# A fused convolution and two-layer network on one core: channels laid out over partitions, so that VectorE turns 32x32 blocks in place of TensorE's transposes

## The chip, the cores and the metric

The kernel runs on one core of a Trainium2 chip. The metric is the device time of one execution in microseconds (us), as the median of several runs. TensorE is called PE here, VectorE DVE, ScalarE ACT, GpSimd POOL, and SyncE SP, as the profile calls them.

## What is computed

```python
# x: 4 x 4096 x 192, weight_gen: 4 x 4096 x 8 x 7, w_in: 192 x 2048, w_out: 2048 x 192
w = softmax(weight_gen, axis=-1)                    # 7 taps for each token and each of 8 heads
x_unf = windows of 7 tokens (the token and the 6 before it, zeros before a sequence's start)
y = einsum('bshk,bskhg->bshg', w, x_unf)            # 24 channels per head, 192 in all
h = y.reshape(16384, 192) @ w_in
g = where(h >= 1, h, where(h <= -1, 0, (h + 1)**2 / 4))
out = g @ w_out
```

## The kernel before

**Tiling.** The 16384 tokens are cut into 128 runs of 128 tokens, one run on each partition. A group is 4 tokens of each run, 512 tokens; there are 32 groups, in 16 pairs (`pair`, `b`). The group of two buffers is `b`. The first pair and the last are written out, the 14 between are a loop.

**The convolution.** For a group, `softmax` makes the taps `tap_w` in six DVE steps with an exponential on ACT between the second and the third, and `convolve` makes 7 products and 6 sums of 768 elements on each partition into `conv`. For the first group DVE convolves, for the others POOL, two groups ahead of PE's use. 64 of the 192 channels are written twice (line 350), so that the second transpose gives them in both halves of the partitions.

**The turn.** PE needs channels on partitions. `turn(pair, b, part)` (line 598) transposes the next group's `conv` into a PSUM slot with four products by the identity; part 0 is channels 0 to 127, part 1 the other 64, twice. ACT copies a turned part out rounded to fp32r (`xt_high`, `xt_rest`), and DVE subtracts the rounded one from the slot (`xt_low`, lower half of `xt_rest`). `TURN_AFTER` says after which of the 16 tiles of a group the parts of the next one are turned.

**The network.** A group has 16 tiles `n` of 128 hidden units. `hidden` (line 617) adds up five products of 512 columns in one of four PSUM slots: the weights and the activations are both split into a rounded and a remaining part. ACT makes `half_relu` and `square`, DVE the `gate`, ACT rounds it (`gate_high`), DVE makes the rest (`gate_low`), and three tiles later (`LAG`) PE's `outputs` (line 637) adds eight products to the accumulators `acc`. At tile 2 of the next group the accumulators are copied, summed and stored.

**The start.** The weights are loaded in four chunks and split by ACT (`in_high`, `out_high`) and DVE (`in_low`, `out_low`), partly before the loop, partly at the tiles of the first group named in `LOWS_AFTER`.

**What sets the order.** All of it is written out by hand: each engine runs its own list in order and waits on semaphores. SP issues nearly all transfers: for each group `store` (two groups back), then `reload` (two groups ahead, once `conv` of the group that used the buffer is done).

Of the kernel before, what the change touches and what calls it, by code (L numbers as in the profile page):

```python
# [19 lines left out]
P = 128  # L20
SLOTS = 4
# [5 lines left out]
OUT_HIGHS_AFTER = {2: 2, 4: 3}  # L27
# [4 lines left out]
TURN_AFTER = (3, 8)  # L32
FIRST_TURNS_AFTER = ((12, 14), (5, 10))
EVICT_AT = 2

# [4 lines left out]
def build(nc, x, weight_gen, w_in, w_out, out):  # L40
# [5 lines left out]
    RUN = B * S // P  # L46
    TOK = 4
    GT = TOK * P
    GROUPS = RUN // TOK
    PAIRS = GROUPS // 2  # L50
    PAD = K - 1
    R = D - P
    HK = H * K
    CT = NT // W_CHUNKS
    CW = FF // W_CHUNKS
    USES = NT + 2
    SEQ_PARTS = S // RUN
    assert R == 64 and (2 * USES) % SLOTS == 0 and NT % W_CHUNKS == 0 and GROUPS % 2 == 0

    x_runs = x.rearrange("b s d -> (b s d)").rearrange("(p r) -> p r", p=P)  # L60
    w_runs = weight_gen.rearrange("b s h k -> (b s h k)").rearrange("(p r) -> p r", p=P)
    out_runs = out.rearrange("t d -> (t d)").rearrange("(p r) -> p r", p=P)
    w_out_tiles = w_out.rearrange("(n p) d -> p n d", p=P)

    with ExitStack() as ctx:
# [7 lines left out]
        x_in = [sb(f"x_in{b}", [P, TOK + PAD, D]) for b in range(2)]  # L73
        gen_in = [sb(f"gen_in{b}", [P, TOK * H, K]) for b in range(2)]
        tap_w = [sb(f"tap_w{b}", [P, TOK, H, K]) for b in range(2)]
        gen_max = sb("gen_max", [P, TOK * H])
        gen_shift = sb("gen_shift", [P, TOK * H, K])
        gen_exp = sb("gen_exp", [P, TOK * H, K])
        gen_sum = sb("gen_sum", [P, TOK * H])
        gen_sum_eps = sb("gen_sum_eps", [P, TOK * H])  # L80
        gen_inv = sb("gen_inv", [P, TOK * H])

        conv = [sb(f"conv{b}", [P, TOK, D + R]) for b in range(2)]
        tap = [sb(f"tap{b}", [P, TOK, D]) for b in range(3)]
        ident = sb("ident", [P, P])
# [27 lines left out]
        in_loaded = [sem(f"in_loaded{c}") for c in range(W_CHUNKS)]  # L113
        out_w_loaded = [sem(f"out_w_loaded{c}") for c in range(W_CHUNKS)]
        x_padded = sem("x_padded")
        ident_done = sem("ident_done")
# [12 lines left out]
        turned = sem("turned")  # L129
        turned_high_done = sem("turned_high_done")  # L130
        turned_low_done = sem("turned_low_done")
# [34 lines left out]
        def turn_after(pair, b):  # L166
            if is_first(pair):
                return FIRST_TURNS_AFTER[b]
            return () if b == 1 and is_last(pair) else TURN_AFTER

        def uses(pair, b):
            order = []
            for n in range(NT):
                order.append(("tile", n))
                order += [("turn", part) for part, at in enumerate(turn_after(pair, b)) if at == n]
            return order

        def tile_slot(pair, b, n):
            return slot[(USES * b + uses(pair, b).index(("tile", n))) % SLOTS]

        def turn_slot(pair, b, part):

            if b == 0 and is_first(pair):
                return slot[2 + part]
            pair, b = before(pair, b)
            return slot[(USES * b + uses(pair, b).index(("turn", part))) % SLOTS]
# [15 lines left out]
        def slot_free(eng, pair, b, use):  # L202


            held = uses(pair, b).index(use) - SLOTS
            if held < 0 and b == 0 and is_first(pair):
                if held >= -2:
                    eng.wait_ge(turned_low_done, held + 3)
                return
            if held < 0:  # L210
                pair, b = before(pair, b)
            kind, k = uses(pair, b)[held]
            if kind == "tile":
                wait(eng, gate_low_done, pair, 2 * NT, NT * b + k + 1)
            else:
                wait(eng, turned_low_done, pair, 4, 2 * (b + 1) + k + 1)

# [6 lines left out]
        def is_edge(pair):  # L224
            return isinstance(pair, int) and pair == 1

        EDGE_X = 1 + 2 * B
        block = ctx.enter_context(nc.Block())

        @block.sync  # L230
        def _(sp):
            def load_gen(pair, b):
                at = (at_pair(pair) * 2 + b) * (TOK * HK)
                sp.dma_start(gen_in[b][:].rearrange("p t k -> p (t k)"),
                             w_runs[:, bass.ds(at, TOK * HK)]).then_inc(gen_loaded[b], 16)

            def load_x(pair, b):

                at = ((at_pair(pair) * 2 + b) * TOK - PAD) * D
                sp.dma_start(x_in[b][:].rearrange("p t d -> p (t d)"),  # L240
                             x_runs[:, bass.ds(at, (TOK + PAD) * D)]).then_inc(x_loaded[b], 16)

            def load_edge_x(b):

                before = PAD - b * TOK
                half = SEQ_PARTS // 2
                flat = x_in[b][:].rearrange("p t d -> p (t d)")
                sp.dma_start(flat[:, before * D:], x_runs[:, 0:(TOK + PAD - before) * D]
                             ).then_inc(x_loaded[b], 16)
                for s in range(B):  # L250
# [22 lines left out]

            load_x(0, 0)
            load_in(0)
            load_in(1)
            load_out(0)
            load_gen(0, 1)
            load_in(2)
# [405 lines left out]
```

## Time and profile before

| what | value |
|---|---|
| median of 3 runs | 1238.05 us (1237.85 to 1238.25) |
| the profiled execution | 1238.25 us, its span 1236.5 us |
| granted TensorE clock, mean | 0.999 of full speed |
| PE busy | 1208.8 us, 98% |
| DVE, ACT, POOL busy | 819.2, 897.5, 696.5 us |
| HBM traffic | 38.77 MB read, 12.58 MB written |

The span is the time from the first to the last instruction; the execution takes 1.75 us more. Busy shares are averages over a start in which PE has little to do and 31 groups that are alike.

### The profile page before, as it was taken

To read this page: it belongs to the slowest core of one execution; us is meant where nothing else is said; L and a number is where in the kernel's file an instruction comes from. 1 tells how busy PE (TensorE), PEld (TensorE's weight loads), DVE (VectorE), ACT (ScalarE), POOL (GpSimd) and SP (SyncE) were. 2 spreads that over 40 slices of the span, in tenths; PEclk is the share of its full clock that TensorE was granted. 3 is DMA by queue.
4 is the path that set the end of the run, shared out by engine and by line. 5 is a ranking of instruction groups with operands and counts; after the bars stand their busy time and mean duration, and the time that the engine had idled before them with its cause. 6 is when DMAs were issued, how large, how long until landed. Compare 5 with 4: busy or idle time off the path is not lost.

```text
span 1236.5 us, 21147 instructions
## 1 busy us (share of the span) xinstructions
PE 1208.8 (98%) x6932; PEld 1092.3 (88%) x6932; DVE 819.2 (66%) x1434; ACT 897.5 (73%) x1773; POOL 696.5 (56%) x450
## 2 busy tenths in 40 slices
PE   3899999999999999999999999999999999999998
PEld 3789999999999999999999999999999999999997
DVE  7966666666666666666666666666666666666665
ACT  4677777777777777777777777777777777777776
POOL 1975775546765456765557755567654567655500
PEclk9999999999999999999999999999999999999999
DMA  7111101111011111011111011110011110110000
GB/s 225 36 50 49 39 11 48 48 49 48 13 35 48 48 48 48 0 48 48 48 48 38 10 48 48 48 48 16 32 48 48 48 48 0 48 48 13 14 14 13
DMA packets 17667, 51.60 MB, mean 42 GB/s; under 512 B 2040, under 2 KB 8308, under 8 KB 17648
## 3 DMA queue, kind: packets, MB, share of 16 engines
q1 hardware_dynamic: 17504, 51.25, 12.7%
q8 instruction: 10, 0.16, 0.1%
q10 hardware_dynamic: 144, 0.11, 0.0%
q14 instruction: 9, 0.07, 0.0%
HBM read 38.77 MB, written 12.58 MB: 42 GB/s over the span
## 4 chain that ended last, share of the span: by engine, by line
PE 93%; POOL 4%; DVE 2%; DMA 0%; ACT 0%; issue 0%; POOLq 0%; DVEq 0%
PE slot L617 46%; PE acc L637 44%; PE slot L598 2%; POOL tap L329 2%; POOL conv L348 1%; DMA gen_in<-in_weight_gen 0%; DVE tap L329 0%; POOL tap L348 0%; POOL x_in L373 0%; POOL conv L352 0%; DVE conv L348 0%; POOL conv L329 0%; POOL conv L350 0%; DVE gate_low L510 0%; ACT gate_high L407 0%
## 5 line engine op out<-in xcount | busy, mean ns | idle before, releaser
L637 PE MATMUL acc<-out_parts,gate_high 128*128 128x384 f32 x2048 | 616.0, 357 | 4.9 <-DVE gate_low L510 4.8
L510 DVE TENSOR_TENSOR gate_low<-slot,gate_high 128x512 fp32r<-128x512 f32 x512 | 353.5, 690 | 400.5 <-ACT gate_high L407 400.3
L396 ACT ACTIVATE half_relu<-slot 128x512 f32<-128x512 f32 x512 | 307.7, 601 | 289.0 <-PE slot L617 288.9
L637 PE MATMUL acc<-out_parts,gate_low 128*128 128x192 f32 x2048 | 513.3, 251 | 0.5 <-DVE gate_low L510 0.5
L637 PEld LDWEIGHTS acc<-out_parts,gate_high 128*128 128x128 f32 x2048 | 384.4, 188 | 26.8 <-DVE gate_low L510 8.1
L637 PEld LDWEIGHTS acc<-out_parts,gate_low 128*128 128x128 f32 x2048 | 389.8, 190 | 17.8 <-DVE gate_low L510 0.7
L504 DVE SCALAR_TENSOR_TENSOR slot<-slot,square 128x512 f32<-128x512 f32 x512 | 352.8, 689 | 0.1
L402 ACT ACTIVATE square<-half_relu 128x512 f32<-128x512 f32 x512 | 325.2, 635 | 0.0
L407 ACT ACTIVATE gate_high<-slot 128x512 fp32r<-128x512 f32 x512 | 304.0, 594 | 27.9 <-DVE slot L504 27.7
L329 POOL TENSOR_TENSOR conv<-x_in,tap_w 128x768 f32<-128x768 f32 x31 | 47.9, 1546 | 460.0 <-DVE tap_w L494 459.9
L329 POOL TENSOR_TENSOR tap<-x_in,tap_w 128x768 f32<-128x768 f32 x186 | 288.8, 1560 | 0.0
L348 POOL TENSOR_TENSOR conv<-conv,tap 128x768 f32<-128x768 f32 x124 | 230.6, 1860 | 0.0
L617 PE MATMUL slot<-xt_high,in_main_high 128*128 128x512 f32 x512 | 211.6, 413 | 0.7 <-DVE in_rest_low L540 0.3
L617 PE MATMUL slot<-xt_low,in_main_high 128*128 128x512 f32 x512 | 202.1, 395 | 0.0
L617 PE MATMUL slot<-xt_rest,in_rest_high 128*128 128x512 f32 x512 | 201.3, 393 | 0.2 <-DVE xt_rest L523 0.2
L617 PE MATMUL slot<-xt_high,in_main_low 128*128 128x512 f32 x512 | 201.1, 393 | 0.0
L617 PE MATMUL slot<-xt_rest,in_rest_low 128*128 128x512 f32 x512 | 199.1, 389 | 0.0
L617 PEld LDWEIGHTS slot<-xt_rest,in_rest_low 128*128 128x128 f32 x512 | 96.2, 188 | 23.0
L617 PEld LDWEIGHTS slot<-xt_rest,in_rest_high 128*128 128x128 f32 x512 | 96.0, 188 | 22.7 <-DVE xt_rest L523 0.5
L617 PEld LDWEIGHTS slot<-xt_low,in_main_high 128*128 128x128 f32 x512 | 96.1, 188 | 21.6 <-DVE xt_low L519 0.5
L617 PEld LDWEIGHTS slot<-xt_high,in_main_low 128*128 128x128 f32 x512 | 97.7, 191 | 0.1
L617 PEld LDWEIGHTS slot<-xt_high,in_main_high 128*128 128x128 f32 x512 | 96.2, 188 | 1.5 <-issue 0.8
(41 smaller groups left out, 492.7 us busy)
## 6 DMA issues: line engine op xcount, KB each, us to landing
x_in<-in_x SPq DMA_DIRECT2D x30, 960.0 KB, 5.1
out<-out_sb SPq DMA_DIRECT2D x32, 384.0 KB, 2.5
gen_in<-in_weight_gen SPq DMA_DIRECT2D x31, 112.0 KB, 2.3
out_raw<-in_moe_w_out SPq DMA_DIRECT2D x4, 384.0 KB, 10.6
in_main<-in_moe_w_in SPq DMA_DIRECT2D x4, 256.0 KB, 6.1
in_rest<-in_moe_w_in SPq DMA_DIRECT2D x8, 128.0 KB, 6.5
x_in<-in_x SPq DMA_DIRECT2D x1, 768.0 KB, 4.1
x_in<-in_x SPq DMA_DIRECT2D x1, 384.0 KB, 3.4
```

What stands on the lines that cost most here:

```text
L329: ops.tensor_tensor(dst[:, :, 0:D].rearrange("p t (h c) -> p t h c", h=H), x_in[b][:, k:k + TOK, :].rearrange("p t (h c) -> p t h c", h=H) ...
L348: ops.tensor_tensor(to, conv[b][:, :, 0:D], tap[k % 3][:], ALU.add).then_inc(step_sem, 1)
L396: nc.scalar.activation(half_relu[n % 2][:], tile_slot(pair, b, n)[:], ACT.Relu, scale=0.5, bias=0.5).then_inc(relu_done, 1)
L402: nc.scalar.activation(square[n % 2][:], half_relu[n % 2][:], ACT.Square).then_inc(square_done, 1)
L407: nc.scalar.activation(gate_high[n % 4][:], tile_slot(pair, b, n)[:], ACT.Copy).then_inc(gate_high_done, 1)
L504: nc.vector.scalar_tensor_tensor(h[:], h[:], 1.0, square[n % 2][:], ALU.max, ALU.min).then_inc(gate_done, 1)
L510: nc.vector.tensor_tensor(gate_low[n % 4][:], tile_slot(pair, b, n)[:], gate_high[n % 4][:].bitcast(F32), ALU.subtract).then_inc(gate_low_ ...
L598: ins = nc.tensor.transpose(dst[:, i * P:(i + 1) * P], conv[b][:, i, part * P:(part + 1) * P], ident[:])
L617: ins = nc.tensor.matmul(tile_slot(pair, b, n)[:], w[:, units], xt[b][:], start=(j == 0), stop=(j == len(products) - 1))
L637: ins = nc.tensor.matmul(dst, stationary, moving, start=(n == 0 and j == 0), stop=(n == NT - 1 and j == 1))
```

## The change

The tokens are now 32 runs ("lanes") of 512 tokens, and a partition is one lane and one quarter of the channels: quarter `q` of lane `r` is partition 32`q` + `r`. A group is 16 tokens of each lane. A partition holds 48 of the 192 channels: 32 "main" ones and 16 "rest". DVE's 32x32 block transpose (`turn_main`) of the main ones gives 4 x 32 channels on 128 partitions. Of the rest, ACT writes the rounded part and POOL (for the first group DVE) what remains beside it, in `rest_parts`, and a second block transpose (`turn_rest`) gives both on 128 partitions. `main_turn` is split by ACT and POOL into `xt_high` and `xt_low`. `rest_turn` is copied to `xt_rest` by a transfer from SBUF to SBUF that SP issues (for the first group by ACT). No channel is written twice any more. The rows of `w_in` are loaded in the order of the new partitions.

Loads change their shape. `x` and `weight_gen` are read in four transfers each, one for a quarter, in runs of 48 floats (192 B) and 14 floats (56 B), where before a partition's 7,680 B and 896 B were contiguous in HBM; at the start the `x` of the first group is loaded from ACT's queue. ACT's splits of the later weight chunks move into the first group (`HIGHS_AFTER`), PE's slots are used by tiles alone, and the second to fifth product of a hidden tile stand in another order.

```diff
-OUT_HIGHS_AFTER = {2: 2, 4: 3}
+HIGHS_AFTER = {1: ("out", 1), 3: ("in", 6), 4: ("in", 7), 5: ("out", 2), 7: ("out", 3)}
-TURN_AFTER = (3, 8)
-FIRST_TURNS_AFTER = ((12, 14), (5, 10))
+MAIN_AFTER, REST_AFTER = 3, 8
+FIRST_MAIN_AFTER, FIRST_REST_AFTER = (11, 7), (13, 10)
...
+        def load_gen(eng, pair, b, q):
+            lanes = slice(q * LANES, (q + 1) * LANES)
+            eng.dma_start(gen_in[b][lanes].rearrange("p (t h) k -> p t (h k)", h=HQ),
+                          w_quads[q][:, bass.ds(group_at(pair, b) * STEP, STEP), :]
+                          ).then_inc(gen_loaded[b], 16)
+        def load_x(eng, pair, b, q):
+            lanes = slice(q * LANES, (q + 1) * LANES)
+            eng.dma_start(x_in[b][lanes],
+                          x_quads[q][:, bass.ds(group_at(pair, b) * STEP - PAD, STEP + PAD), :]
+                          ).then_inc(x_loaded[b], 16)
+        def load_main(eng, c):
+            eng.dma_start(in_main[:, cols], w_in_quads[:, 0:MAIN, cols]).then_inc(main_loaded[c], 16)
...
+            def copy_rest(pair, b):
+                wait(sp, rest_turned, pair, 2, b + 1)
+                sp.dma_start(xt_rest[b][:].bitcast(F32), rest_turn[:]).then_inc(xt_rest_copied, 16)
             def body(pair):
                 for b in range(2):
                     if not is_first(pair):
                         store(pair - 1, b)
                     if not is_last(pair):
                         reload(pair + 1, b)
+                    if has_next(pair, b):
+                        copy_rest(*after(pair, b))
...
-            ops.tensor_tensor(conv[b][:, :, D:D + R], tap[K % 3][:, :, P:D],
-                              tap[(K - 1) % 3][:, :, P:D], ALU.add).then_inc(step_sem, 1)
...
+            def lows(pair, b):
+                wait(pool, rest_high_done, pair, 2, b + 1)
+                rest_low(nc.gpsimd, b).then_inc(rest_low_done, 1)
+                wait(pool, xt_high_done, pair, 2, b + 1)
+                wait(pool, hidden_done, pair, 2 * NT, NT * (b - 1))
+                main_low(nc.gpsimd, b).then_inc(xt_low_done, 1)
...
                         convolve(pool, nc.gpsimd, pair + 1, b)
+                        lows(pair + 1, b)
...
-            def turned_top(pair, b, part):
-                wait(act, turned, pair, 4, 2 * b + part + 1)
-                dst = (xt_high, xt_rest)[part][b]
-                nc.scalar.activation(dst[:], turn_slot(pair, b, part)[:], ACT.Copy
+            def rest_high(pair, b):
+                nc.scalar.activation(rest_parts[:, :, 0:REST], conv[b][:, :, MAIN:CH], ACT.Copy
+            def main_high(pair, b):
+                nc.scalar.activation(xt_high[b][:], main_turn[:], ACT.Copy).then_inc(xt_high_done, 1)
...
+            for half in range(4):
+                in_high(half)
             out_high(0)
-            turned_top(0, 0, 0)
-            turned_top(0, 0, 1)
+            rest_high(0, 0)
+            main_high(0, 0)
+            act.wait_ge(rest_turned, 1)
+            nc.scalar.activation(xt_rest[0][:], rest_turn[:], ACT.Copy).then_inc(first_xt_rest_done, 1)
             exponent(0, 1)
-            out_high(1)
+            in_high(4)
+            in_high(5)
...
-            def turned_rest(pair, b, part):
-                    nc.vector.tensor_tensor(xt_low[b][:], src[:], xt_high[b][:].bitcast(F32),
-                                            ALU.subtract).then_inc(turned_low_done, 1)
+            def turn_main(pair, b):
+                nc.vector.transpose(main_turn[:], by_block(conv[b][:])[:, :, :, 0:MAIN]
+            def turn_rest(pair, b):
+                nc.vector.transpose(rest_turn[:], by_block(rest_parts[:].bitcast(F32))
...
             convolve(dve, nc.vector, 0, 0)
+            dve.wait_ge(rest_high_done, 1)
+            rest_low(nc.vector, 0).then_inc(first_rest_low_done, 1)
+            turn_main(0, 0)
+            turn_rest(0, 0)
+            dve.wait_ge(xt_high_done, 1)
+            main_low(nc.vector, 0).then_inc(first_xt_low_done, 1)
             in_low(0)
             in_low(1)
             softmax(0, 1, 1)
-            turned_rest(0, 0, 0)
-            turned_rest(0, 0, 1)
...
-            def turn(pair, b, part):
-                for i in range(TOK):
-                    ins = nc.tensor.transpose(dst[:, i * P:(i + 1) * P],
-                                              conv[b][:, i, part * P:(part + 1) * P], ident[:])
```

PE's list, at a tile of the looped groups after which a part was turned. Before:

```order
L617 MATMUL slot<-xt_rest,in_rest_high 128x512
L617 MATMUL slot<-xt_rest,in_rest_low 128x512
L598 MATMUL slot<-ident,conv 128x128 x4
L149 REGISTER_ALU
L637 MATMUL acc<-out_parts,gate_high 128x384
```

The same place in the changed kernel:

```order
L689 MATMUL slot<-xt_high,in_main_high 128x512
L689 MATMUL slot<-xt_low,in_main_high 128x512
L689 MATMUL slot<-xt_rest,in_rest_high 128x512
L689 MATMUL slot<-xt_high,in_main_low 128x512
L689 MATMUL slot<-xt_rest,in_rest_low 128x512
L173 REGISTER_ALU
L709 MATMUL acc<-out_parts,gate_low 128x192
```

The four products of line 598 are gone from it, and the five of the tile stand in another order.

SP's list at the start of the program (shapes are those of the SBUF side). Before:

```order
L240 DMA x_in<-in_x 128x1920
L264 DMA in_main<-in_moe_w_in 128x512
L267 DMA in_rest<-in_moe_w_in 64x512 x2
L264 DMA in_main<-in_moe_w_in 128x512
L267 DMA in_rest<-in_moe_w_in 64x512 x2
L271 DMA out_raw<-in_moe_w_out 128x4x192
L234 DMA gen_in<-in_weight_gen 128x224
L264 DMA in_main<-in_moe_w_in 128x512
```

In the changed kernel:

```order
L233 DMA gen_in<-in_weight_gen 32x16x14 x4
L246 DMA in_main<-in_moe_w_in 128x1x512
L253 DMA in_rest<-in_moe_w_in 16x512 x4
L275 DMA out_raw<-in_moe_w_out 128x4x192
L246 DMA in_main<-in_moe_w_in 128x1x512
L253 DMA in_rest<-in_moe_w_in 16x512 x8
L233 DMA gen_in<-in_weight_gen 32x16x14 x4
L240 DMA x_in<-in_x 32x22x48 x4
L246 DMA in_main<-in_moe_w_in 128x1x512
L253 DMA in_rest<-in_moe_w_in 16x1024 x8
```

The third chunk of `in_main` now stands behind the whole of the second group's `gen_in` and `x_in`, eight transfers of short runs.

## Rows read from the trace of the kernel before

**Rows 1.** The page: busy time, and the chain that ended last.

```profile
PE 1208.8 (98%) x6932; PEld 1092.3 (88%) x6932; DVE 819.2 (66%) x1434; ACT 897.5 (73%) x1773; POOL 696.5 (56%) x450
PE slot L617 46%; PE acc L637 44%; PE slot L598 2%; POOL tap L329 2%; POOL conv L348 1%; DMA gen_in<-in_weight_gen 0%; DVE tap L329 0%; POOL tap L348 0%; POOL x_in L373 0%; POOL conv L352 0%; DVE conv L348 0%; POOL conv L329 0%; POOL conv L350 0%; DVE gate_low L510 0%; ACT gate_high L407 0%
```

**Rows 2.** PE's timeline in two groups: start, duration (us), line, operation.

```profile
507.37 0.41 PE L617 MATMUL slot<-xt_high,in_main_high 128*128 128x512 f32 x1
...
521.09 0.41 PE L617 MATMUL slot<-xt_high,in_main_high 128*128 128x512 f32 x1
...
524.59 0.60 PE L598 MATMUL slot<-ident,conv 128*128 128x128 f32 x4
...
562.07 0.60 PE L598 MATMUL slot<-ident,conv 128*128 128x128 f32 x4
```

**Rows 3.** Groups by form: xcount | busy us, mean ns | idle before.

```profile
L348 POOL TENSOR_TENSOR conv<-conv,tap 128x768 f32<-128x768 f32 x124 | 230.6, 1860 | 0.0
L598 PE MATMUL slot<-ident,conv 128*128 128x128 f32 x256 | 38.3, 273 | 1.5 <-POOL conv L352 0.8 <-DVE conv L352 0.5 <-DVE gate_low L510 0.2
L350 POOL TENSOR_TENSOR conv<-tap 128x256 f32<-128x256 f32 x31 | 22.8, 737 | 2.4
L519 DVE TENSOR_TENSOR xt_low<-slot,xt_high 128x512 fp32r<-128x512 f32 x32 | 21.8, 680 | 0.0
L414 ACT ACTIVATE xt_high<-slot 128x512 fp32r<-128x512 f32 x32 | 18.9, 590 | 1.6 <-PE slot L598 1.6
```

**Rows 4.** POOL's and DVE's timeline about one group's convolution.

```profile
500.21 1.55 POOL L329 TENSOR_TENSOR conv<-x_in,tap_w 128x768 f32<-128x768 f32 x1 [15.39 <-DVE tap_w L494]
520.59 1.86 POOL L352 TENSOR_TENSOR conv<-tap 128x768 f32<-128x768 f32 x1
528.10 0.68 DVE L519 TENSOR_TENSOR xt_low<-slot,xt_high 128x512 fp32r<-128x512 f32 x1
```

**Rows 5.** DVE's and PE's timeline for the tile of 507.37 us.

```profile
512.15 0.69 DVE L510 TENSOR_TENSOR gate_low<-slot,gate_high 128x512 fp32r<-128x512 f32 x1 [0.99 <-ACT gate_high L407]
515.40 0.33 PE L637 MATMUL acc<-out_parts,gate_high 128*128 128x384 f32 x1
```

**Rows 6.** The start: timeline of DVE and PE.

```profile
6.27 0.39 DVE L479 TENSOR_REDUCE gen_max<-gen_in 128x32 f32<-128x224 f32 x1 [6.27 <-DMA gen_in<-in_weight_gen]
9.13 0.96 DVE L329 TENSOR_TENSOR conv<-x_in,tap_w 128x768 f32<-128x768 f32 x1
20.02 0.95 DVE L352 TENSOR_TENSOR conv<-tap 128x768 f32<-128x768 f32 x1
24.18 0.40 PE L617 MATMUL slot<-xt_rest,in_rest_low 128*128 128x512 f32 x1
```

**Rows 7.** Windows of start and first group: busy us, PEclk, DMA share, GB/s.

```profile
0.00:22.36 22.36, 5.31 (x28) 4.91 (x28) 15.29 (x23) 7.65 (x13) 0.78 (x8) 1.00 0.92 264
22.36:65.21 42.85, 37.09 (x192) 30.13 (x193) 39.35 (x55) 28.78 (x54) 38.24 (x24) 1.00 0.18 51
```

**Rows 8.** DVE's timeline in the first group, beside POOL at work.

```profile
36.08 0.37 DVE L479 TENSOR_REDUCE gen_max<-gen_in 128x32 f32<-128x224 f32 x1
48.11 1.64 DVE L494 TENSOR_TENSOR tap_w<-gen_exp,gen_inv 128x224 f32<-128x224 f32 x1
50.88 1.82 DVE L540 TENSOR_TENSOR in_main_low<-in_main,in_main_high 128x512 fp32r<-128x512 f32 x1
```

**Rows 9.** DMA, windows 0:40, 531:531.4, 1235:1236.4: packets, MB, 16 engines' share.

```profile
q10 hardware_dynamic: 144, 0.11, 0.9%
...
q1 hardware_dynamic: 5, 0.00, 0.7%
...
q1 hardware_dynamic: 79, 0.19, 35.5%
```

**Rows 10.** DMA issues: KB each, median us from issue to landing.

```profile
out<-out_sb SPq DMA_DIRECT2D x32, 384.0 KB, 2.5
gen_in<-in_weight_gen SPq DMA_DIRECT2D x31, 112.0 KB, 2.3
```

More of the change, by code:

```diff
@@ L162, in is_last, with main_after, rest_after, has_next @@
             return isinstance(pair, int) and pair == PAIRS - 1
[L166 to L186, printed above, removed]
+        def main_after(pair, b):
+            return FIRST_MAIN_AFTER[b] if is_first(pair) else MAIN_AFTER
+        def rest_after(pair, b):
+            return FIRST_REST_AFTER[b] if is_first(pair) else REST_AFTER
+        def has_next(pair, b):
+            return not (b == 1 and is_last(pair))
+        def tile_slot(n):
+            return slot[n % SLOTS]
         def before(pair, b):
@@ L200, in wait_conv @@
                 wait(eng, conv_done, pair, 2, at)
[L202 to L216, printed above, removed]
         def at_pair(pair):
@@ L230, in _ @@
         @block.sync
         def _(sp):
[L232 to L241, printed above, removed]
@@ new lines, in wait_rest_low, with wait_xt_low, rest_low @@
+        def wait_rest_low(eng, pair, b):
+            if b == 0 and is_first(pair):
+                eng.wait_ge(first_rest_low_done, 1)
+            else:
+                wait(eng, rest_low_done, pair, 2, b)
+        def wait_xt_low(eng, pair, b):
+            if b == 0 and is_first(pair):
+                eng.wait_ge(first_xt_low_done, 1)
+            else:
+                wait(eng, xt_low_done, pair, 2, b)
+        def rest_low(ops, b):
+            return ops.tensor_tensor(rest_parts[:, :, REST:2 * REST], conv[b][:, :, MAIN:CH],
+                                     rest_parts[:, :, 0:REST].bitcast(F32), ALU.subtract)
@@ L423, in take_cross, with in_high @@
                                          ).then_inc(cross_copied, 1)
[L425 to L426 removed]
+            for q in range(QUADS):
+                load_x(act, 0, 0, q)
+            load_rest(act, 0, 0)
             exponent(0, 0)
[L429 removed]
+            def in_high(half):
+                c, rest = divmod(half, 2)
                 cols = slice(c * CW, (c + 1) * CW)
[L431 to L433 removed]
+                if rest:
+                    act.wait_ge(rest_loaded[min(c, 2)], 16 * 2 * QUADS)
+                else:
+                    act.wait_ge(main_loaded[c], 16)
+                raw, high = ((in_main, in_main_high), (in_rest, in_rest_high))[rest]
+                nc.scalar.activation(high[:, cols], raw[:, cols], ACT.Copy).then_inc(in_high_done, 1)
             def out_high(c):
@@ L588, in _ @@
         def _(pe):
-            def turn(pair, b, part):
-                if not (b == 0 and is_first(pair)):
-                    slot_free(pe, *before(pair, b), ("turn", part))
-                if part == 0:
-                    wait_conv(pe, pair, b)
-                dst = turn_slot(pair, b, part)
-                for i in range(TOK):
-                    ins = nc.tensor.transpose(dst[:, i * P:(i + 1) * P],
-                                              conv[b][:, i, part * P:(part + 1) * P], ident[:])
-                ins.then_inc(turned, 1)
```

303 lines of the change are left out of this document (173 added, 130 removed).

## The prediction

> **What bounds the kernel now.** I read the busy times and the chain of waits first [rows 1]: PE is busy for 1208.8 us of a span of 1236.5, and the chain runs almost wholly through its products, 46% in the hidden tiles, 44% in the outputs and 2% in the transposes of line 598. Then the timeline of PE far from both ends [rows 2]: two hidden tiles six apart start at 507.37 and 521.09 us, so a tile takes 13.72 / 6 = 2.287 us, and the same transposes come back after 562.07 - 524.59 = 37.48 us. Sixteen tiles are 36.59 us, so the two turned parts cost a group 0.89 us of PE's time. The view by groups gives 256 transposes of 273 ns, 38.3 us in all [rows 3]; they overlap, so 0.89 a group is the price on the path.
>
> The start has other limits. The first tile ends at about 24.6 us (24.18 + 0.40), behind the load of `gen_in` (the softmax waits for it until 6.27), the softmax (convolution from 9.13) and the convolution (until 20.97) [rows 6]. The DMA engines are 92% busy there at 264 GB/s [rows 7]. The first group then takes 42.85 us, though its three missing outputs make it shorter than the others: DVE is busy for 39.35 of them [rows 7], since it splits the weights. So the time is: 65.21 us to the end of the first group, 30 groups of 37.48, the last, which turns nothing, of 36.59, and 10.3 us that remain of the span behind it. The profiled execution took 1238.25 us, 1.75 more than its span and 0.2 more than the median of 1238.05, which is nothing here: a difference of 0.2% is about what a measurement of this kernel can tell from none.
>
> **Steady groups: what is removed.** Without line 598 a group is 36.59 us. 30 x 0.89 = 26.7 us.
>
> **Steady groups: what is added.** DVE loses two subtractions of 512 columns a group at 0.68 us [rows 3] and gains two block transposes of 512 columns. No row shows a block transpose. The nearest is the subtraction of as many columns, 0.68; I take 0.7. It may also have to wait for POOL: beside POOL's work DVE's `tap_w` took 1.64 and `in_main_low` 1.82 us, while `gen_max` took 0.37 [rows 8]; the usual `in_main_low` of as many columns would be 0.68, so the wait is up to 1.2 us. `turn_main` falls where POOL is idle, `turn_rest` (tile 8) where POOL convolves. Bounds: 0.4 (the 0.37 of `gen_max`, a DVE row of half the columns) to 4 x 0.68 + 1.2 = 3.9 us, if the turn took four passes. What covers it: DVE is idle 0.99 us in every tile, and the `gate_low` of the tile that started at 507.37 ends at 512.84 while PE uses it at 515.40 [rows 5], 2.56 us later. A turn is free up to 0.99 + 2.56 = 3.5 us.
>
> The Trainium skill (VectorE: DVE Perf Modes, The three transpose paths) gives 311 ns for a 128x128 bf16 transpose on VectorE. Four of these would be an estimated 1.24 us for ours, also under cover; no run here shows it yet.
>
> ACT's two copies of a turned part, 0.59 each [rows 3], become one of 512 and one of 256 columns. POOL loses the doubled channels (0.74) and gains `rest_low` of the same size (0.74) and `main_low` (512 of 768 columns at 1.86, 1.24 us). It is idle 15.39 us before each convolution, waiting for the taps of tile 7 [rows 4]; the lows run at tiles 3 to 5 of that gap. The convolution ended at 522.45 (520.59 + 1.86) and the turn's DVE work began at 528.10 [rows 4]: 5.6 us in hand. I take nothing for all of it.
>
> SP now waits for `rest_turned` (tile 8) before it issues the copy; behind it stand `store` and `reload`. The reload is then issued 11 tiles (25 us) before DVE asks for `gen_in` at tile 3 of the next group. The copy has 8 tiles (18 us) to land; a transfer of 384 KB lands in 2.5 us, one of 112 KB in 2.3 [rows 10], so 2.4 is the copy's. Nothing.
>
> **What a short run costs.** A group's loads are 4 x 32 x 16 = 2048 runs of 56 B and 4 x 32 x 22 = 2816 of 192 B, 4864 packets, 304 for each of 16 engines. Prices from the DMA windows [rows 9]: 5 semaphore packets took 0.7% of 16 x 0.4 us, 9 ns each; those of the 144 of queue 10 that carry 896 B took 0.9% of 16 x 40 us less 16 x 9 ns over 128, 44 ns each; 63 of 3072 B, 35.5% of 16 x 1.4 us less the same, 124 ns each. A line through the last two gives 18 ns for 192 B and 13 for 56 B, 15 in the mean: the low end. The high end is a flat 44. I take 35, nearer to the flat one, for short reads scattered in HBM. A group's loads are then 10.6 us of a 36.6 us group: hidden.
>
> The Trainium skill (DMA: Bandwidth & Descriptors, Specifications) asks for at least 512 B and says that below it an engine reads, modifies and writes. It speaks against this change and gives no price; no packet of data under 512 B is in this trace.
>
> **The start.** `gen_in` and `x_in` of the first group come on two queues that share the engines. A transfer's fixed part is about 2 us (2.3 less 8 x 44 ns) and the first issue stands at 0.75. `gen_in` lands at 0.75 + 2 + 256 x 0.035 = 11.7 us; the softmax's 2.86 us (9.13 - 6.27) put the convolution at 14.6, **+5.5**. Two halves in place of the last sum and the doubled channels: -0.25. Then DVE does `rest_low` (0.4), both turns (1.4) and `main_low` (0.7), `in_low` (1.2), and the first tile ends about 4.5 us after the convolution where it was 3.6: **+0.9**. ACT has two splits of 0.6 before the loop instead of one: I take **+0.8**, in_main and in_rest together being longer than the one they replace. These need the third weight chunk: behind 2.75 + 10.6 us stand 1.44 MB of weights at 264 GB/s (5.5), the second group's loads (10.6) and 0.79 MB more (3.0), 32.4 us, then 1.2 of splitting: **+1.5** beyond what ACT would have reached. The first copy has only tiles 13 to 16: DVE ends a gate 3.8 us after its tile began (512.15 less its 0.99 us of idle time, against 507.37 [rows 5]), then come the turn (0.7) and issue and transfer (0.6 + 2.4), 7.5 us. PE wants it in the third product of the third tile on, 3 x 2.287 + 0.46 = 7.3. In the first group DVE runs late by a split or so: **+1.0**. The two turns of the first group go: -0.9. Together +8.6.
>
> **Sum:** 65.2 + 8.6 + 31 x 36.59 + 10.3 = 1218.4, plus 1.75: **1220 us**.
>
> With 608 short packets per engine on the way to the loop, each ns of price is 0.6 us once ACT waits for weights: 15 ns gives 1213, 44 ns gives 1226.
>
> **Rivals.**
>
> *Late weights, slower than before.* From 31 ns on, the start costs 608 t - 12.5 us (t in us), and it eats the 26.7 saved at t = 65 ns. The mean over all startup packets of this trace is no guide, since they are long. At 90 ns, twice the 896 B row, the time is 1254; against it stands that price falls with size between the three rows. A packet above 120 ns would also fill a group. Chance 0.08.
>
> *Fewer engines.* `load_main` and `store` now have a side whose outermost dimension is 4. If that decides how many engines share a transfer, a store's 32 packets per engine instead of 8 take 24 x 124 ns = 3.0 us more on the last store, and three chunks of `in_main` at 24 more packets of about 90 ns (between the 44 and 124 rows) are 6.5 us later; both add: 1220 + 9.5 = 1229 us. Chance 0.27.
>
> The Trainium skill (DMA: Bandwidth & Descriptors, Why a DMA increments its semaphore by 16 and not by 1) states this rule: the largest number up to 16 that divides both sides' slowest dimension. Every large transfer of this trace has 64 or 128 rows on both sides, so no row bears it out or refutes it.
>
> *DVE becomes the bound.* If a turn beside POOL takes the 3.9 us of the upper bound, PE waits 0.4 us in 31 groups: 1232. Slower than before from 4.2 us on. Chance 0.05.
>
> *The saving is smaller because PE waited for something else anyway.* Against: in the rows of the page PE is at 98%, and the removed products stand between tiles with no gap. That the transposes stay is excluded by PE's list. Chance 0.02, 1236.
>
> **Chances.** The likeliest, short packets between 15 and 50 ns, all 16 engines: 0.58, with 1211 to 1229. Faster by over 0.2% is that, fewer engines and most of the DVE case: 0.89. Slower: late weights and a piece of the DVE case, 0.09. Same: 0.02. The range goes from 1210 (low price, nothing lost at the first copy) to 1234 (fewer engines and a price of 43 ns).
>
> **What the next profile would show.** Right: no PE idle time inside steady groups, tiles of 2.287 us, 36.6 a group; DVE's transposes near 0.7 us, the second up to 1.9; POOL's wait for the taps about 13 us; the first tile ending near 30 us. Wrong: PE waiting for `xt_rest` each group (the copy is late), DVE `gen_max` waiting for `gen_in` in the loop (short packets over 65 ns), ACT waiting for `in_main` before the loop for more than 5 us (price, or fewer engines), `gate_low` named as PE's releaser (DVE).

## The result and the profile after

The changed kernel takes 1222.03 us (median; 1221.9 to 1223.1) against 1238.13 measured beside it (1237.85 to 1238.25), a ratio of 0.9872 (0.9855 to 0.9889). It is 16.1 us faster, 1.3%, and 2 us from the predicted 1220. The agreement is partly luck: three errors of 3 to 7 us cancel in it, as the sections below take apart.

The page of the changed kernel, in the same views as [rows 1]: the span, the busy times, and (the fourth line from its section 4) the chain that ended last.

```profile
span 1220.2 us, 21278 instructions
...
PE 1185.1 (97%) x6676; PEld 1066.4 (87%) x6676; DVE 841.3 (69%) x1436; ACT 901.4 (74%) x1774; POOL 731.9 (60%) x473
...
PE 93%; DVE 2%; SPq 2%; ACT 1%; DMA 1%; issue 0%; DVEq 0%
```

PE has 256 instructions fewer (6932 to 6676), the transposes of line 598. It is still the bound, at 97%, but SP's issuing now has 2% of the chain, at the start. The new loads read less (24.62 MB instead of 38.77) in many more packets (171,875 instead of 17,667); the main DMA queue's share of the 16 engines rose from 12.7% to 18.5%.

PE's timeline, the first product of chosen tiles (start, duration, line, operation), as in [rows 2]: the first tile of group 1, the third product of its first tile, the first tile of group 2, tiles 1 to 4 of a later group (583.91 to 590.92), the first tile of the last group, and the last tile of all.

```profile
66.65 0.41 PE L689 MATMUL slot<-xt_high,in_main_high 128*128 128x512 f32 x1
...
67.65 0.50 PE L689 MATMUL slot<-xt_rest,in_rest_high 128*128 128x512 f32 x1 [0.35 <-DMA xt_rest<-rest_turn]
...
104.11 0.41 PE L689 MATMUL slot<-xt_high,in_main_high 128*128 128x512 f32 x1
...
583.91 0.41 PE L689 MATMUL slot<-xt_high,in_main_high 128*128 128x512 f32 x1
...
586.20 0.41 PE L689 MATMUL slot<-xt_high,in_main_high 128*128 128x512 f32 x1
...
588.50 0.39 PE L689 MATMUL slot<-xt_high,in_main_high 128*128 128x512 f32 x1
...
590.92 0.41 PE L689 MATMUL slot<-xt_high,in_main_high 128*128 128x512 f32 x1
...
1169.42 0.41 PE L689 MATMUL slot<-xt_high,in_main_high 128*128 128x512 f32 x1
...
1203.91 0.41 PE L689 MATMUL slot<-xt_high,in_main_high 128*128 128x512 f32 x1
```

The first tiles of group 1, of group 2 and of the last group, and the last tile, in the kernel before, which [rows 2] do not hold:

```profile
65.21 0.41 PE L617 MATMUL slot<-xt_high,in_main_high 128*128 128x512 f32 x1
...
103.87 0.41 PE L617 MATMUL slot<-xt_high,in_main_high 128*128 128x512 f32 x1
...
1191.76 0.41 PE L617 MATMUL slot<-xt_high,in_main_high 128*128 128x512 f32 x1
...
1226.27 0.41 PE L617 MATMUL slot<-xt_high,in_main_high 128*128 128x512 f32 x1
```

With the two spans these starts cut the 16.3 us of span into four parts:

| part | before | after | difference | predicted |
|---|---|---|---|---|
| to the first tile of group 1 | 65.21 | 66.65 | +1.4 | +8.6 |
| 30 groups, per group | 37.55 | 36.76 | -23.8 in all | -26.7 |
| first to last tile of the last group | 34.51 | 34.49 | 0.0 | 0 |
| start of the last tile to the end of the span | 10.23 | 16.29 | +6.1 | 0 |

The predicted +8.6 holds 1.0 for the first copy of `rest_turn`; what that copy cost was paid in group 1. Group 1 is longer than the 29 behind it in both kernels: 38.66 us against 37.51 before, 37.45 against 36.73 after. Before, one of its turns waited 0.8 us for POOL's convolution [rows 3]; after, its first tile waits for the copy.

The rows 583.91 to 590.92 show a loss inside the groups: tiles come every 2.29 and 2.30 us, and then one takes 2.42. The views by form and by wait tell more: the groups that answer to [rows 3], and the waits of POOL, PE's loader and SP (us in all, times, longest).

```profile
L586 DVE STREAM_TRANSPOSE main_turn<-conv 128x512 f32<-128x512 f32 x32 | 22.5, 702 | 0.0
L596 DVE STREAM_TRANSPOSE rest_turn<-rest_parts 128x512 f32<-128x512 f32 x32 | 22.4, 701 | 0.0
```

```profile
POOL conv L352 <- DVE tap_w L559: 187.3, 29, 6.5
POOL rest_parts L397 <- ACT rest_parts L461: 158.5, 31, 8.2
PEld acc L709 <- DVE out_sb L603: 8.5, 28, 0.3
PEld slot L689 <- DMA xt_rest<-rest_turn: 0.8, 1, 0.8
SPq L331 <- DMA out<-out_sb: 7.9, 1, 7.9
```

DVE's transpose is as quick as forecast, the copy of `rest_turn` is waited for once, at the first copy, and SP's last wait, for the last store, is 7.9 us. In the kernel before it was

```profile
SPq L310 <- DMA out<-out_sb: 2.0, 1, 2.0
```

### The profile page after: what moved, and what is told of

It reads as the page before. It is cut to its first block, busy times and chain, and to the rows that moved or that the text cites. A ratio compares the mean times of both kernels' runs of the same rounds, so it can differ in the third digit from the quotient of the medians.

```text
span 1220.2 us, 21278 instructions
## 1 busy us (share of the span) xinstructions
PE 1185.1 (97%) x6676; PEld 1066.4 (87%) x6676; DVE 841.3 (69%) x1436; ACT 901.4 (74%) x1774; POOL 731.9 (60%) x473
## 2 busy tenths in 40 slices
DMA packets 171875, 45.59 MB, mean 37 GB/s; under 512 B 160848, under 2 KB 162896, under 8 KB 171856
## 3 DMA queue, kind: packets, MB, share of 16 engines
q1 hardware_dynamic: 168848, 44.68, 18.5%
HBM read 24.62 MB, written 12.58 MB: 30 GB/s over the span
## 4 chain that ended last, share of the span: by engine, by line
PE 93%; DVE 2%; SPq 2%; ACT 1%; DMA 1%; issue 0%; DVEq 0%
PE slot L689 48%; PE acc L709 46%; DVE slot L569 1%; SPq L253 1%; DMA in_rest<-in_moe_w_in 1%; DVE gate_low L575 1%; SPq L233 1%; ACT gate_high L451 0%; DVE out_parts L620 0%; SPq L240 0%; DMA xt_rest<-rest_turn 0%; SPq L246 0%; ACT square L446 0%; DVE gen_sum_eps L552 0%; DVE gen_shift L546 0%
## 5 line engine op out<-in xcount | busy, mean ns | idle before, releaser
L397 POOL TENSOR_TENSOR rest_parts<-conv,rest_parts 128x256 fp32r<-128x256 f32 x31 | 22.8, 737 | 158.5 <-ACT rest_parts L461 158.5
```

What stands on the lines that cost most here:

```text
L397: return ops.tensor_tensor(rest_parts[:, :, REST:2 * REST], conv[b][:, :, MAIN:CH], rest_parts[:, :, 0:REST].bitcast(F32), ALU.subtract)
```

## The experiments

Three questions stood after the result: what made the tail 6 us longer, what took back 3 us of the steady saving, and why the start cost so little. Where two medians of different kernels are subtracted below, the changed kernel's 1222.03 is the base unless said otherwise. The diffs are cut: the semaphore counts that go with an edit are left out.

### The last store

The store's HBM side is now `j r g e`, with 4 outermost. The view of the DMA queues over the last stretch (packets, MB, share of 16 engines), 1226:1236.5 of the kernel before and 1210:1220.2 of the changed one, each with just one store in it:

```profile
q1 hardware_dynamic: 144, 0.39, 9.6%
```

```profile
q1 hardware_dynamic: 132, 0.39, 14.6%
```

Both carry 128 data packets of 3072 B. The others are semaphore packets, 16 before and 4 now: four engines took part. Their work is 0.146 x 16 x 10.2 = 23.8 us, 186 ns a packet, and 32 packets on each of four engines are 6.0 us. The data packets ran from 1212.50 to 1219.43, so 3.4 were under way at a time in the mean; before, they ran from 1234.50 to 1235.63, at 124 ns a packet 14 at a time. The Trainium skill (DMA: Bandwidth & Descriptors, Why a DMA increments its semaphore by 16 and not by 1) says that each engine taking part posts one semaphore write and that their number is the largest up to 16 that divides both sides' slowest dimension; the trace agrees, with 4 and 16.

**The store in four transfers of 32 partitions**, in the changed kernel:

```diff
-                sp.dma_start(out_steps[:, :, bass.ds(group_at(pair, b), 1), :],
-                             out_sb[b][:].rearrange("p t d -> p (t d)"))
+                for j in range(STEP // TOK):
+                    lanes = slice(j * LANES, (j + 1) * LANES)
+                    sp.dma_start(out_steps[j][:, bass.ds(group_at(pair, b), 1), :],
+                                 out_sb[b][lanes].rearrange("p t d -> p (t d)"))
```

> The changed kernel with each store of 384 KB issued as four transfers of 32 lanes (one for each of the four steps j) instead of one transfer whose HBM side has 4 as its outermost dimension. Theory (that outermost 4 lets only four DMA engines share the store): the last store lands in about 3 us instead of 8.7, plus up to 1.5 us for three more issues; the time falls by 4 to 6 us, to 1216 to 1218. Rival (the store is slow because its rows are scattered in HBM): nothing changes in the rows, so the time stays at 1222.

1216.81 us (1216.66 to 1217.05), 5.2 less. From the start of the last tile to the end of the span it is now 11.00 us in place of 16.29 (10.23 before the change); what is left of the difference, 0.8, is about what SP needs for four issues in place of one (1.71 us against 0.54). A packet is no quicker in the four transfers (208 ns in the mean); more of them run at a time. SP's last wait:

```profile
SPq L333 <- DMA out<-out_sb: 1.4, 1, 1.4
```

**The same HBM pattern alone, in the kernel before** (it writes each token's output to another place of `out`):

```diff
+                rows = out_runs.rearrange("(r j) e -> j r e", j=4)
-                sp.dma_start(out_runs[:, bass.ds(at, TOK * D)],
+                sp.dma_start(rows[:, :, bass.ds(at, TOK * D)],
```

> The kernel before with its store written with an HBM side of 4 x 32 rows, the order of the changed kernel's store, same rows of 3072 B and the same count; each output row goes to another place of the output, so the output is permuted. Theory (four engines): the last store lasts 6 us longer and the time is 1244. Rival (the changed kernel's end is longer for another reason): 1238.

1244.12 us (1243.94 to 1244.38), 1.005 of the kernel before (1.0033 to 1.0066), 6.0 slower. Its groups take 37.55 us as before, and the stretch behind the last tile's start grew from 10.23 to 16.32. So the pattern alone accounts for the whole tail. It also holds up what queues behind it, as the landing times of `gen_in` (last number) show; here they cost nothing, since the loads have a group's time in hand.

```profile
gen_in<-in_weight_gen SPq DMA_DIRECT2D x31, 112.0 KB, 8.4
```

In the kernel before that was 2.3 [rows 10].

### The steady groups

DVE adds up the accumulators (`out_sb`) at the first tiles of a group, and PE's first `outputs` of that group, at tile 3, needs them free. DVE's and PE's timeline there:

```profile
588.69 0.69 DVE L575 TENSOR_TENSOR gate_low<-slot,gate_high 128x512 fp32r<-128x512 f32 x1 [0.99 <-ACT gate_high L451]
589.29 1.14 DVE L603 TENSOR_TENSOR out_sb<-acc,out_cross 128x192 f32<-128x192 f32 x4
...
589.70 0.44 PE L709 MATMUL acc<-out_parts,gate_high 128*128 128x384 f32 x1
```

The sums stand behind a `gate_low` on DVE and begin at 589.29, and the first product into `acc` follows at 589.70, about when the first of the four sums is done; this tile is the one of 2.42 us, 0.13 longer than its neighbours. In the kernel before, the four transposes after tile 3 stood between the hidden tile and these products, 0.44 us in which the wait was hidden.

**Four products of 128 columns put back after tile 3**, on the identity, into the slot of the next tile, their results unused:

```diff
                         hidden(pair, b, n)
+                        if n == 3 and has_next(pair, b) and not (b == 0 and is_first(pair)):
+                            wait(pe, gate_low_done, pair, 2 * NT, NT * b + n + 1 - SLOTS + 1)
+                            for i in range(TOK):
+                                nc.tensor.transpose(tile_slot(n + 1)[:, i * P:(i + 1) * P], warm[:], warm[:])
```

> The changed kernel with four transposes of a constant 128x128 tile put back on PE behind hidden tile 3, where the first turned part stood, in 30 groups; their result is overwritten. Theory (in the kernel before these products hid part of PE's wait for the accumulators to be summed, so that only part of their 0.43 us was a price): a group grows by 0.43 less the wait of 0.15 to 0.2, so 30 x 0.25 = 7.5 us, to 1229 to 1230. Rival (the wait has nothing to do with it): 30 x 0.43 = 12.9 us, to 1235.

1231.72 us (1231.49 to 1231.81), 9.7 more. This lies between the two values forecast, 1229 to 1230 and 1235, nearer to the theory's. **The same after tile 8** (`n == 8`), where the old kernel turned its second part:

> The same four transposes behind hidden tile 8, where PE waits for nobody. Both theories: 30 x 0.43 = 12.9 us, to 1235. The difference to the run with them behind tile 3 is the wait that they cover there: 5 us by the theory, 0 by the rival.

1235.38 us (1235.30 to 1237.02), 13.35 more. The profiled execution is the one of 1237.02; what it took longer lies ahead of group 1, which starts there at 68.30. The waits of PE's loader in the first of the two:

```profile
PEld acc L713 <- DVE gate_low L579: 8.5, 4, 6.4
PEld slot L693 <- ACT xt_high L471: 1.7, 1, 1.7
```

and in the second:

```profile
PEld acc L713 <- DVE out_sb L607: 8.5, 28, 0.3
```

At tile 3 the wait for `out_sb` is gone; at tile 8 it stands as in the changed kernel. The two differ by 3.66 us, less than the 5 I expected. Per group, between the first tiles of group 1 and of the last, they take 37.085 and 37.202 us against 36.759. So four products cost 0.443 where they cover nothing, and 0.326 at tile 3: the cover was worth **0.117 us a group**, 3.5 in all. The wait's row says 8.5 / 28 = 0.30 a time; that is time of the loader, most of it under a running product.

**The sums ahead of the gate on DVE**, nothing else changed:

```diff
-                        if n > 0:
-                            gate_rest(pair, b, n - 1)
-                        ...
                         if n == EVICT_AT and not (b == 0 and is_first(pair)):
                             sum_outputs(*before(pair, b))
+                        if n > 0:
+                            gate_rest(pair, b, n - 1)
+                        ...
```

> The changed kernel with DVE's four sums of the accumulators ahead of gate_low at tile 2 of a group instead of behind it. Theory (PE waits 0.1 to 0.2 us in each group for the sums, since the transposes that covered them are gone): the sums come 0.35 us earlier, the wait goes, and the time falls by 3 to 4.5 us, to 1218. Rival (the run with products behind tile 3 was shorter for another reason): 1222, or more if gate_low then comes late.

1218.45 us (1218.30 to 1218.55), 3.6 less; groups of 36.642 us, 0.117 less, and PE's waits name `out_sb` no more. **The same edit in the kernel before**, as a control, since there the transposes should cover the wait:

> The same exchange in the kernel before, as a control. Theory (there the transposes cover the sums in 31 groups of 32): within 1 us of 1238. Rival (an earlier sum helps whatever stands on PE): 1234.

1237.81 us (1237.64 to 1238.15), 0.9998 of the kernel before (0.9989 to 1.0008): no change, and its groups take 37.55 us as before. That settles it. The price of the two turned parts, 2 x 0.443 = 0.887, less the lost cover of 0.117 is 0.77 a group, where 37.55 - 36.76 = 0.79 was measured.

### The start

ACT's timeline, its last DMA waits before the loop and its first `half_relu`:

```profile
27.54 0.63 ACT L490 ACTIVATE in_main_high<-in_main 128x512 fp32r<-128x512 f32 x1 [1.79 <-DMA in_main<-in_moe_w_in]
29.71 0.63 ACT L490 ACTIVATE in_rest_high<-in_rest 128x512 fp32r<-128x512 f32 x1 [1.53 <-DMA in_rest<-in_moe_w_in]
30.25 0.58 ACT L440 ACTIVATE half_relu<-slot 128x512 f32<-128x512 f32 x1
```

In the kernel before the first `half_relu` was at

```profile
25.28 0.58 ACT L396 ACTIVATE half_relu<-slot 128x512 f32<-128x512 f32 x1
```

so ACT entered the loop 5.0 us late, and 3.3 of it are the waits for the third weight chunk. But PE began its first tile at 22.73 (before: 22.36) and group 1 only 1.4 us later than before: the first group won back 3.5. The chain that ended last runs through SP's issues up to the last part of `in_rest`'s third chunk, and then through its load:

```profile
22.22 7.47 DMA in_rest<-in_moe_w_in
```

So three things stand ahead of this wait: the issues of so many transfers, the short runs, and how fast the weights land. **`in_main` in four transfers of 32 rows** asks whether the wait is another case of four engines:

```diff
-            eng.dma_start(in_main[:, cols], w_in_quads[:, 0:MAIN, cols])
+            for q in range(QUADS):
+                eng.dma_start(in_main[q * LANES:(q + 1) * LANES, cols], w_in_quads[q][0:MAIN, cols])
```

> The changed kernel with each chunk of in_main loaded in four transfers of 32 rows instead of one whose HBM side is 4 x 32. Theory (four engines carry it alone, and they hold up what is queued behind on them): chunk 3 of the weights, which ACT got 9 us after its issue, lands 4 us or less after it; eight more issues stand ahead of it on SP, some 4 us, so ACT's wait stays about as it is and the time is 1221 to 1224. Rival (the transfers are late only because SP issues them late): landing after issue does not change and the time grows by the issues, 1225 to 1227.

1219.74 us (1219.62 to 1219.93), 2.3 less and outside the 1221 to 1224 that I expected: I had left ACT's wait as it was, and it went. The issues and landings of the changed kernel:

```profile
out_raw<-in_moe_w_out SPq DMA_DIRECT2D x4, 384.0 KB, 9.7
...
in_rest<-in_moe_w_in SPq DMA_DIRECT2D x8, 64.0 KB, 5.4
```

and of this one, where both waits of ACT are gone and the first `half_relu` starts at 26.69:

```profile
out_raw<-in_moe_w_out SPq DMA_DIRECT2D x4, 384.0 KB, 4.8
...
in_rest<-in_moe_w_in SPq DMA_DIRECT2D x8, 64.0 KB, 2.8
```

The transfers *behind* `in_main` land in half the time after their issue although they weren't touched. They are there earlier in the trace's own time too: ACT's split of the first chunk of `in_rest` starts at 10.27 instead of 13.09, that of the second at 14.05 instead of 17.68. So `in_main`, on its four engines, had held up their parts on these engines. Group 1 starts at 64.20 instead of 66.65; the first group, from PE's first tile on, takes 41.48 us instead of 43.92.

**The third chunk issued ahead of the second group's short loads:**

```diff
+            load_main(sp, 2)
+            for half in range(2):
+                load_rest(sp, half, 2)
             for q in range(QUADS):
                 load_gen(sp, 0, 1, q)
             for q in range(QUADS):
                 load_x(sp, 0, 1, q)
-            load_main(sp, 2)
-            for half in range(2):
-                load_rest(sp, half, 2)
```

> The changed kernel with the third chunk of in_main and the rest of in_rest loaded ahead of the second group's gen_in and x_in on SP. Theory (ACT's waits for the third chunk, 1.8 and 1.5 us before its first relu, hold up the start): they go, the first relu comes 3 us earlier, and the time falls by 1.5 to 3 us, to 1219 to 1220.5, since DVE bounds the rest of the first group. Rival (DVE would have been late by as much anyway): 1222.

1221.45 us (1220.93 to 1221.52), 0.6 less. ACT's splits no longer wait and its first `half_relu` is at 28.29, but PE's first tile starts at 24.32 in place of 22.73: ACT waited 11.0 us instead of 7.9 for the first two chunks and came to `rest_parts` at 22.12 instead of 20.49. The first group takes 41.46 us. So the wait went as wholly as with `in_main` in four parts, and most of it came back ahead of the first tile; the expectation of 1.5 to 3 was wrong. Why the first two chunks land later was not tested.

**Long rows in the first pair**: its `x` and `weight_gen` are read as 4,224 B and 896 B contiguous on each partition (the first two groups then compute on other values).

```diff
+            if is_first(pair):
+                eng.dma_start(gen_in[b][lanes].rearrange("p a k -> p (a k)"),
+                              w_flat[:, q * STEP * HQ * K:(q + 1) * STEP * HQ * K])
+                return
...
```

> The changed kernel with the loads of x and weight_gen of the first two groups taken as one contiguous run for each partition, as many bytes and as many transfers; these two groups compute on other values than the reference's. It prices the short runs at the start. By the prediction (35 ns a packet, 600 packets an engine) 8 us of the start would go: 1214. By the trace of the changed kernel (15 to 20 ns a packet; first convolution at 9.5 us against 9.1) ACT's wait for chunk 3 shrinks by 3 us at most: 1219 to 1221.

1219.60 us (1218.94 to 1221.00), 2.4 less: all the short runs of the start cost together 2.4 us, with a wider spread than the other runs have. By the prediction's price of 35 ns it would have been 1214. PE's first tile starts at 21.81, 0.9 earlier, and the first group takes 41.44 us. These three edits differ, and each brings the first group from 43.92 to 41.4 or 41.5: each takes away by itself all that PE felt of ACT's late start. Their gains need not add, no run has two of them, and the wait can't be put down to one of the three causes. The price itself can be read in the loop, where nothing else moves. The changed kernel's DMA queues over 614:617:

```profile
q1 hardware_dynamic: 2326, 0.41, 74.3%
```

0.743 x 16 x 3.0 us over 2326 packets is **15.3 ns** each, for a mix of 56 and 192 B (176 B in the mean). And the start agrees: DVE's timeline,

```profile
6.63 0.39 DVE L544 TENSOR_REDUCE gen_max<-gen_in 128x32 f32<-128x224 f32 x1 [6.63 <-DMA gen_in<-in_weight_gen]
...
9.49 0.96 DVE L352 TENSOR_TENSOR conv<-x_in,tap_w 128x768 f32<-128x768 f32 x1
```

has the softmax at 6.63 where the prediction's own formula gives 0.75 + 2 + 256 x 0.0153 = 6.67, and the convolution 2.86 behind it.

### The copy of the rest

**By ACT instead of by a transfer**, at tile 9:

```diff
-                    if has_next(pair, b):
-                        copy_rest(*after(pair, b))
...
+                        if n == rest_after(pair, b) + 1 and has_next(pair, b):
+                            take_rest(*after(pair, b))
```

> The changed kernel with rest_turn copied to xt_rest by ACT (0.63 us, at the tile behind the turn) instead of by a transfer from SBUF to SBUF, in all groups. Theory (the transfer is hidden in all groups but the second, where PE waits 0.8 us for it, and ACT has room): 1221 to 1222. Rival (ACT, 74% busy, makes its copy at the cost of relu and gate, and PE waits in each group): over 1225.

1221.56 us (1221.33 to 1222.75), 0.9869 (0.9853 to 0.9886), too near the changed kernel's to tell from it. Group 1 takes 36.79 us instead of 37.45, the groups behind it 36.73 as before. So the first copy by transfer cost PE 0.65 us, of which the row of 67.65 shows 0.35 as idle time just before the product; all later ones were hidden, and so are ACT's.

### The repairs together

**Store and `in_main` in four transfers each:**

> Both transfers spread: the stores and the chunks of in_main of the changed kernel each issued as four transfers of 32 rows. The two act in different places, so their gains should add: 1222.0 - 5.2 - 2.3 = 1214.5. If the start's gain depended on the slow stores it would be less.

1214.68 us (1214.64 to 1214.71); 1222.03 - 5.2 - 2.3 = 1214.5. **With the sums first and the copy by ACT too:**

> The changed kernel with the four-part stores, the four-part in_main, the sums ahead of gate_low and the copy to xt_rest by ACT. If all gains add (5.2, 2.3, 3.7, 0.5 to 1.1): 1210. If two of them answer to the same wait: 1212 to 1214.

1210.00 us (1209.87 to 1210.08), 0.9773 of the kernel before (0.9757 to 0.9789). It is the best version here, with groups of 36.62 us and 10.99 us behind the last tile's start. The repairs add up. Of the 4.7 us between the two runs the sums make 3.5 and the copy about 1.1: with the earlier start group 1 took 37.69 us, and with ACT's copy it takes 36.62.

## Why the prediction held, and where it did not

The direction and the main mechanism were right; the number was right because errors cancelled.

- **"Without line 598 a group is 36.59 us. 30 x 0.89 = 26.7 us."** Mis-sized by 2.9 us. The price of the two turns was right (2 x 0.443 = 0.887, by the tile 8 run), but a product that is removed can have covered a wait of the next one. I had looked for covers on DVE, ACT and POOL, and none on PE itself. That cover is 3.5 us. The late first copy adds 0.65 in group 1, and 1.15 by which group 1 had been longer than the others before went with the change; together 3.0. With the sums first, the groups behind group 1 take 36.62 us, 0.03 above the predicted 36.59.
- **"No PE idle time inside steady groups, tiles of 2.287 us."** Wrong at tile 3 of every group (2.42 us), for that reason.
- **The price of a short packet, 35 ns.** Wrong by more than two; the low end, 15 by the line through the trace's own rows, was right (15.3). I chose "nearer to the flat one, for short reads scattered in HBM", for which no row spoke. This took the convolution's delay from +5.5 to +0.36. For 15 ns the prediction's text gives 1213; with 2.9 lost in the groups and 6.1 in the tail that is 1222.
- **The start, "+8.6", measured +1.4.** The convolution makes 5.1 of the error. From it to PE's first tile nothing was lost, where I had +0.65. For ACT's lateness I had "+0.8" and "+1.5", and the first group is 2.45 longer than in the three runs that take the wait away. That size was right, but the reasons were not the ones of the sum alone: four engines for `in_main` were as needed for it as the short runs. ACT was 5.0 us late at its first `half_relu`, and PE felt half of it. Without the wait the first group takes 41.5, 1.4 less than the 42.85 before, where I had -0.9 for its turns; the other 0.5 was not traced. The +1.0 for the first copy fell into group 1, as 0.65.
- **The likeliest case assumed all 16 engines; the rival "Fewer engines" is what happened.** It was given 0.27. Its last store was priced at +3.0 with 124 ns a packet and measured +6.1: 32 packets of 186 ns against 8 of 124 make 5.0 of it. Why a packet takes 186 was not tested. Its weights were priced at +6.5, and splitting them gave back 2.3. Its sum of 9.5 compares with the 7.35 that the two repairs gave back together (1222.03 to 1214.68).
- **DVE's turn, 0.7.** 702 and 701 ns, and not longer beside POOL's convolution. The rival in which DVE becomes the bound did not occur. The Trainium skill's page (VectorE: DVE Perf Modes, The three transpose paths), from which I had an estimated 1.24 us, was further off than the subtraction of as many columns.
- **POOL's wait for the taps "about 13 us".** Wrong in place and size: it is at most 6.5, since POOL now waits before that for ACT's `rest_parts` (up to 8.2) and `xt_high` (up to 1.7). Its slack was there and nothing came of it, as forecast.
- **SP, reload and copy: nothing.** Right: no wait for `gen_in` or `x_in` in the loop. The first copy was late, as forecast: it cost 0.65 us, by the run with ACT's copy, where I had +1.0.

## What to carry to other kernels

When a layout change puts a small number outermost on either side of a transfer, count the semaphore packets of that transfer in the trace: with 4 instead of 16 the last store and everything queued behind such a load paid here, and splitting it into as many transfers gave it back. When several causes stand ahead of one wait, an edit that takes the wait away doesn't show that its cause was the only one: try the others alone too. When work is taken off the bounding engine, ask which wait of that same engine it had covered, at the instruction just behind it; an order that is free in one version costs in the next. Price an unseen operation or packet by the line through the rows at hand, and leave it only for a row that speaks against it.

## What the runs showed of the hardware

**`gen_shift`, a DVE operation with two inputs in SBUF, stretched beside POOL; the block transpose didn't.** DVE's and then POOL's timeline of the changed kernel:

```profile
595.00 1.38 DVE L546 TENSOR_TENSOR gen_shift<-gen_in,gen_max 128x224 f32<-128x224 f32 x1
...
603.76 0.70 DVE L596 STREAM_TRANSPOSE rest_turn<-rest_parts 128x512 f32<-128x512 f32 x1
```

```profile
594.84 1.30 POOL L401 TENSOR_TENSOR xt_low<-main_turn,xt_high 128x512 fp32r<-128x512 f32 x1 [1.52 <-ACT xt_high L467]
...
602.55 1.54 POOL L352 TENSOR_TENSOR conv<-x_in,tap_w 128x768 f32<-128x768 f32 x1 [6.42 <-DVE tap_w L559]
```

`gen_shift` ends just after POOL's `xt_low`; over all groups its mean rose from 430 to 1331 ns. The transpose of one input runs while POOL is at its products (the next one follows at 604.05) and keeps its 0.70 us; over all groups `rest_turn` took 0.67 to 0.70. Neither costs time here.

**TensorE's clock fell at the start.** Windows of the changed kernel: busy us of PE, PEld, DVE, ACT, POOL, the granted clock, DMA share, GB/s.

```profile
20.00:22.00 2.00, 0.85 (x6) 0.66 (x5) 1.97 (x5) 0.42 (x1) 0.34 (x1) 1.00 0.63 99
...
22.00:24.00 2.00, 1.03 (x3) 0.52 (x3) 1.90 (x5) 1.23 (x2) 0.00 (x0) 0.92 1.05 181
24.00:26.00 2.00, 2.00 (x6) 1.44 (x5) 1.97 (x5) 0.39 (x1) 0.00 (x0) 0.50 1.10 112
...
30.00:32.00 2.00, 0.00 (x0) 0.00 (x0) 0.48 (x1) 1.94 (x4) 2.00 (x2) 1.00 0.70 148
34.00:36.00 2.00, 2.00 (x9) 2.00 (x8) 1.93 (x4) 2.00 (x5) 2.00 (x2) 0.50 0.53 72
```

0.50 is the lower level, 1.2 GHz, and products of 512 columns took 0.63 us there against 0.40. Ahead of the first fall PE was busy for 0.85 us of 20:22 and 1.03 of 22:24; the kernel before, with its transposes in that place, had 1.50 in each and stayed at 1.00, as its windows show:

```profile
20.00:22.00 2.00, 1.50 (x13) 1.19 (x11) 2.00 (x4) 0.42 (x2) 0.00 (x0) 1.00 0.79 241
...
22.00:24.00 2.00, 1.50 (x6) 0.64 (x5) 1.94 (x5) 0.80 (x2) 0.00 (x0) 1.00 0.95 256
```

Ahead of the second fall it was idle from 30 to 32, while ACT was late.

What this cost can be bounded. The run with stores and `in_main` in four parts and the best version differ in the first group by nothing but ACT's copy towards its end, and by the clock; their windows show

```profile
26.00:28.00 2.00, 2.00 (x6) 1.53 (x5) 1.52 (x5) 1.97 (x5) 0.23 (x1) 0.50 0.84 170
```

```profile
26.00:28.00 2.00, 2.00 (x10) 1.58 (x9) 1.48 (x5) 1.97 (x5) 0.27 (x1) 1.00 0.88 197
```

and their group 1 starts at 64.28 and 64.27. The first fall cost nothing that can be seen. The second one, absent with `in_main` in four parts (1.00 in 34:36), comes back at another place in the run that has the stores in four parts too (0.56 and 0.58 in 42:44 and 44:46), and the first group takes 41.46 us as against 41.48. So no part of what splitting `in_main` gained is seen to be clock; a fall at 34 us alone was not tried.
